# Two-stage attention ahead of two feed-forward stages: the order of an attention turn on all engines, and its crossing into the next stage

## What is computed

```python
def sm_attn(qq, kk, vv):
    s = scale * np.matmul(qq, kk.transpose(0, 1, 3, 2))
    s = s - np.max(s, axis=-1, keepdims=True)
    a = np.exp(s)
    a = a / (np.sum(a, axis=-1, keepdims=True) + 1e-09)
    return np.matmul(a, vv)
p_packed = sm_attn(p, k, v)               # q, k, v: (8, 8, 576, 64), p: (8, 8, 32, 64)
out = sm_attn(q, p_packed, p_packed)
x = out.transpose(0, 2, 1, 3).reshape(4608, 512)
h = x @ w_in                              # 512 x 2048
g = (a0 + a1*h + a2*h**2 + a3*h**3) / (1 + |b0|*|h| + |b1|*h**2 + 1e-6)
y = g @ w_out                             # 2048 x 512
h = y @ w_in2                             # 512 x 1024
solu = h * softmax(h); result = layernorm(solu) * g_ln @ w_out2
```

## Time and profile before

| | us |
|---|---|
| median of 3 runs | 1232.92 (1231.55 to 1236.02) |
| the profiled execution | 1235.92 |
| its span, first to last instruction | 1234.1 |
| TensorE busy in the span | 1180.6 (96%) |
| VectorE, ScalarE, GpSimd busy | 1045.4, 832.8, 437.5 |
| data moved, mean rate | 116 MB, 94 GB/s |

### The profile page before, as it was taken

The page is one execution under the profiler, slowest core; times in us unless marked ns, Lnnn a source line. Parts: engine busy times, 40 slices in busy tenths (PEclk is TensorE's granted clock), DMA queues, the critical chain, the costliest instruction groups (busy, mean ns, idle before and its releaser), DMA issues.

```text
span 1234.1 us, 25214 instructions
## 1 busy us (share of the span) xinstructions
PE 1180.6 (96%) x9824; PEld 1049.5 (85%) x9824; DVE 1045.4 (85%) x1621; ACT 832.8 (67%) x1302; POOL 437.5 (35%) x284
## 2 busy tenths in 40 slices
PE   6788887999999999999999999999999999999998
PEld 3455555999999999999999999997788888888887
DVE  3767778999999999999999999988677687776763
ACT  2456559888888888888888888754555454454543
POOL 1333322334343343333433334354434344353300
PEclk8889889999999999999999999999999999999999
DMA  8779975321202212012121121121121121111211
GB/s 286 226 265 348 333 272 217 105 81 38 81 28 64 81 38 80 29 62 81 43 75 37 55 80 37 54 88 44 43 54 49 36 58 43 51 47 38 60 26 35
DMA packets 70758, 116.25 MB, mean 94 GB/s; under 512 B 9728, under 2 KB 40448, under 8 KB 70656
## 3 DMA queue, kind: packets, MB, share of 16 engines
q1 hardware_dynamic: 70656, 114.85, 28.8%
HBM read 74.46 MB, written 40.37 MB: 93 GB/s over the span
## 4 chain that ended last, share of the span: by engine, by line
PE 90%; DVE 5%; issue 3%; ACT 1%; DMA 1%; POOL 0%; SPq 0%; ACTq 0%; DVEq 0%
PE ps_y L73 11%; PE ps_y L75 11%; PE ps_y L74 11%; PE ps_h L73 6%; PE ps_h L75 6%; PE ps_h L74 6%; PE ps_o L73 5%; PE ps_o L75 5%; PE ps_o L74 5%; PE ps_h L1394 4%; PE ps_h L1395 4%; PE ps_h L1396 4%; PE ps_s L381 3%; PE ps_s L394 3%; PE ps_t L1419 2%
## 5 line engine op out<-in xcount | busy, mean ns | idle before, releaser
L1018 POOL TENSOR_TENSOR den<-den,h_abs 128x576 f32<-128x576 f32 x128 | 222.3, 1737 | 401.6 <-ACT den L971 401.6
L73 PE MATMUL ps_y<-g_hi,wout_hi 128*128 128x288 f32 x1024 | 303.6, 297 | 0.0
L74 PE MATMUL ps_y<-g_lo,wout_hi 128*128 128x288 f32 x1024 | 302.6, 295 | 0.0
L75 PE MATMUL ps_y<-g_hi,wout_lo 128*128 128x288 f32 x1024 | 301.6, 295 | 0.0
L75 PEld LDWEIGHTS ps_y<-g_hi,wout_lo 128*128 128x128 f32 x1024 | 193.0, 188 | 0.0
L74 PEld LDWEIGHTS ps_y<-g_lo,wout_hi 128*128 128x128 f32 x1024 | 192.3, 188 | 0.0
L73 PEld LDWEIGHTS ps_y<-g_hi,wout_hi 128*128 128x128 f32 x1024 | 192.1, 188 | 0.3 <-ACT wp_out L530 0.2
L73 PE MATMUL ps_h<-x_hi,wp_hi 128*128 128x288 f32 x512 | 152.3, 298 | 1.3 <-DVE wp_lo L1033 0.8
L74 PE MATMUL ps_h<-x_lo,wp_hi 128*128 128x288 f32 x512 | 151.3, 295 | 0.0
L75 PE MATMUL ps_h<-x_hi,wp_lo 128*128 128x288 f32 x512 | 150.8, 295 | 0.0
L965 ACT ACTIVATE h_abs<-ps_h 128x576 f32<-128x576 f32 x128 | 83.3, 651 | 82.5 <-PE ps_h L75 82.3
(11 more groups left out here) (164 smaller groups left out, 2594.7 us busy)
## 6 DMA issues: line engine op xcount, KB each, us to landing
wp_scratch<-wp_out SPq DMA_DIRECT2D x32, 512.0 KB, 5.3
wp_lo<-wp_scratch SPq DMA_DIRECT2D x32, 512.0 KB, 4.1
k_main<-in_k SPq DMA_DIRECT2D x16, 576.0 KB, 6.7
q_main<-in_q SPq DMA_DIRECT2D x16, 576.0 KB, 6.0
v_main<-in_v SPq DMA_DIRECT2D x16, 576.0 KB, 5.5
y_scratch<-y_out SPq DMA_DIRECT2D x16, 576.0 KB, 3.4
y_lo<-y_scratch SPq DMA_DIRECT2D x36, 256.0 KB, 3.2
out<-result SPq DMA_DIRECT2D x144, 64.0 KB, 1.7
```

The lines of the kernel that those rows point to most:

```text
L73: pe.matmul(out, lh, rh, start=first, stop=False)
L74: pe.matmul(out, lh, rl, start=False, stop=False)
L75: return pe.matmul(out, ll, rh, start=False, stop=last)
L1018: pool.tensor_tensor(den[s % 3][:, :, :], den[s % 3][:, :, :], h_abs[:, :, :], ALU.mult)\
```

## The change

TensorE's turn i becomes: the v products of group i itself in four pieces (20, 16, 20 and 16 products), the two halves of the scores of packed of i+1 behind the first and the second, the two halves of a job behind the third and the fourth, then q's scores of group i-1, packed of i turned, and the queries of i turned. The wait in the middle of q's scores becomes one for the packed tile; the turned packed tile and the ninth query pair move to other PSUM banks (`turn_pack`, `turn_q8`). `job_at` puts job m into turn m + 4, so twelve lie in turns and four in the crossing. The weights get a second staging buffer; two parts are split ahead of the first turn, and in a turn the split stands at the end. SP loads p and k of two groups first, and its turn becomes k, p, weight part, v, a2, job's store, q. kT and the first query buffer change places in SBUF, so that the first wp block waits for the last scores of packed; the tiles of the rational stage's chain are put into other strips. The crossing is written anew on all engines. Removed lines of the loops are left out below where the new ones replace them all.

```diff
-LAST_JOBS = 5
-PAIR_JOBS = 4
+LAST_JOBS = 4
...
-    m = i - QUAD - 1
+    m = i - QUAD
...
+    kT = sb("kT", [P, RUN, DB, PACK])
+    q_main = [sb("q_main0", [P, RUN, DH])]
+    w_stage = [sb("w_stage0", [P, WI]), sbuf.at("w_stage1", [P, WI], sbuf.area - 4 * WI)]
     p_in = [sb(f"p_in{i}", [P, DH]) for i in range(2)]
     v_main = [sb(f"v_main{i}", [P, RUN, DH]) for i in range(2)]
-    kT = sb("kT", [P, RUN, DB, PACK])
+    q_main += [sb("q_main1", [P, RUN, DH])]
...
+    def turn_pack(i):
+        return ps_turn[:, 1, 0:P] if i < GROUPS - 1 else ps_s2[:, 1, HALF + DH:HALF + DH + P]
+    def turn_q8(i):
+        return ps_turn[:, 0, 0:P] if i < GROUPS - 1 else ps_s2[:, 0, HALF:HALF + P]
...
     def parts_at(i):
-        return [i] if i < 5 else [5, 6] if i == 5 else [i + 1] if i < GROUPS - 1 else []
+        return [0, 1] if i < 0 else [i + 2] if i + 2 < 2 * PARTS else []
+    def w_buffer(n):
+        return w_stage[n % 2 if n < 2 * PARTS - 1 else 0]
...
     def next_w(sp, n):
-        sp.wait_ge(w_lo_done, n)
-        load_w(sp, n)
+        after = n + 2 if n < 2 * PARTS - 3 else n + 1
+        if n != 2 * PARTS - 3 and after < 2 * PARTS:
+            sp.wait_ge(w_lo_done, n + 1)
+            load_w(sp, after)
     def sync(sp, coefficients, first_loads):
         first_chunk, first_block, second_block, last_blocks = first_loads
-        load_p(sp, 0)
-        load_k(sp, 0)
-        load_w(sp, 0)
+        for i in range(2):
+            load_p(sp, i)
+            load_k(sp, i)
+        load_v(sp, 0)
         load_q(sp, 0)
-        load_p(sp, 1)
-        load_k(sp, 1)
-        load_v(sp, 0)
+        for n in range(2):
+            load_w(sp, n)
+        sp.wait_ge(kT_ready, 1)
+        load_k(sp, 2)
+        sp.wait_ge(pT_ready, 1)
+        load_p(sp, 2)
+        load_v(sp, 1)
+        sp.wait_ge(kT_ready, 2)
+        load_k(sp, 3)
+        sp.wait_ge(pT_ready, 2)
+        load_p(sp, 3)
         load_q(sp, 1)
+        coefficients(sp)
         for i in range(GROUPS - 1):
-            if i >= 1 and job_at(i - 1) is not None:
-                store_job(sp, job_at(i - 1))
+            if i + 4 < GROUPS:
+                sp.wait_ge(kT_ready, i + 3)
+                load_k(sp, i + 4)
+                sp.wait_ge(pT_ready, i + 3)
+                load_p(sp, i + 4)
+            elif i + 4 == GROUPS:
+                first_chunk(sp)
+            for n in parts_at(i - 1):
+                next_w(sp, n)
             if i + 2 < GROUPS:
-                sp.wait_ge(kT_ready, i + 1)
-                load_k(sp, i + 2)
-                sp.wait_ge(pT_ready, i + 1)
-                load_p(sp, i + 2)
-                sp.wait_ge(qT_done, i + 1)
-                load_q(sp, i + 2)
-            else:
-                first_chunk(sp)
-            if len(parts_at(i)) > 1:
-                next_w(sp, parts_at(i)[1])
-            wait_for(sp, pack_done, i)
-            load_v(sp, i + 1)
-            if i == 0:
-                coefficients(sp)
-            if i + 2 == GROUPS:
+                sp.wait_ge(pack_done, i + 1)
+                load_v(sp, i + 2)
+            if i + 1 == GROUPS - 1:
                 first_block(sp)
             if i >= 2:
                 store_a2(sp, i - 2)
-            if parts_at(i + 1):
-                next_w(sp, parts_at(i + 1)[0])
+            if job_at(i) is not None:
+                store_job(sp, job_at(i))
+            if i + 2 < GROUPS:
+                sp.wait_ge(qT_done, i + 1)
+                load_q(sp, i + 2)
...
+        def pack(pe, i, part):
+            if part == 0:
                 pe.wait_ge(probs1T_ready, i + 1)
                 pe.wait_ge(v_in[i % 2], 16 * (i // 2 + 1))
-                wait_for(pe, scores2_out, i)
-                wait_for(pe, packT4_lo_ready, i)
-            for t in range(half * PAIRS, (half + 1) * PAIRS):
+                wait_for(pe, scores2_out, i - 1)
+                wait_for(pe, packed_ready, i)
+            for t in range((0, 5, 9, 14)[part], (5, 9, 14, 18)[part]):
                 for h in range(GH):
                     mm = pe.matmul(ps_pack[head(h), :], probs1T[head(h), t, :], v_main[i % 2][head(h), t, :],
                                    start=(t == 0), stop=(t == RUN - 1), skip_group_check=True)
-            if half == 1:
+            if part == 3:
...
                 if h == GH // 2:
-                    pe.wait_ge(packT4_lo_ready, i + 1)
+                    pe.wait_ge(*((packed_ready, i + 2) if i < GROUPS - 1 else (packT4_lo_ready, GROUPS)))
...
+        for c in range(2):
+            scores_of_packed(pe, 0, c)
+        turn_last_pair(pe, 0)
+        turn_queries(pe, 0)
+        for c in range(2):
+            scores_of_packed(pe, 1, c)
+        for part in range(4):
+            pack(pe, 0, part)
+        turn_packed(pe, 0)
+        for i in range(1, GROUPS - 1):
+            pack(pe, i, 0)
+            scores_of_packed(pe, i + 1, 0)
+            pack(pe, i, 1)
+            scores_of_packed(pe, i + 1, 1)
+            pack(pe, i, 2)
+            job_block(pe, i, 0)
+            pack(pe, i, 3)
+            job_block(pe, i, 1)
+            scores_of_q(pe, i - 1)
+            turn_packed(pe, i)
+            turn_last_pair(pe, i)
             turn_queries(pe, i)
         last = GROUPS - 1
+        for part in range(3):
+            pack(pe, last, part)
+        pe.wait_ge(exp1_ready, GROUPS)
+        features(pe, 0)
+        pack(pe, last, 3)
+        job_block(pe, last, 0)
+        job_block(pe, last, 1)
+        scores_of_q(pe, last - 1)
+        pe.wait_ge(wp_act_out, 2 * job_at(last) + 1)
+        features(pe, 1)
+        turn_last_pair(pe, last)
+        turn_packed(pe, last)
+        features(pe, 2)
+        turn_queries(pe, last)
+        features(pe, 3)
+        b, c, d, e = range(JOBS - LAST_JOBS, JOBS)
         last_block(pe, b, 0)
+        scores_of_q(pe, last)
         last_block(pe, b, 1)
+        for m in (c, d, e):
             for n in range(2):
                 last_block(pe, m, n)
...
         def turn_packed(pe, i):
             pe.wait_ge(packed_ready, i + 1)
-            pe.transpose(turn_pack, packed.rearrange("p a d -> p (a d)"), ident[:, :]).then_inc(packT_done, 1)
+            if i == GROUPS - 1:
+                pe.wait_ge(scores2_out, GROUPS - 1)
+            else:
+                wait_for(pe, packT4_lo_ready, i)
+                if job_at(i) is not None:
+                    pe.wait_ge(wp_act_out, 2 * job_at(i) + 1)
+            pe.transpose(turn_pack(i), packed.rearrange("p a d -> p (a d)"), ident[:, :]).then_inc(packT_done, 1)
...
-            pe.wait_ge(*((qT8_out, i + 1) if n == 0 else (qT_out, i + 1)))
+            if n == 0:
+                pe.wait_ge(qT8_out, i)
+                pe.wait_ge(packT4_lo_ready, i)
+            else:
+                pe.wait_ge(qT_out, i)
...
+        first_terms(act, 0)
+        for n in parts_at(-1):
+            weights_high(act, n)
         for i in range(GROUPS - 1):
             if i == 3:
                 next_coefficients(act)
+            first_terms(act, i + 1)
             if job_at(i) is not None:
                 job_to_sbuf(act, job_at(i), 0)
                 job_to_sbuf(act, job_at(i), 1)
+            if i == GROUPS - 2:
+                break
+            if i == 0:
+                last_pair_to_sbuf(act, i)
+                qT_to_sbuf(act, i)
+                act.wait_ge(zeros, 1)
+            packT_to_sbuf(act, i)
             if i >= 1:
                 second_terms(act, i - 1)
+                last_pair_to_sbuf(act, i)
+                qT_to_sbuf(act, i)
+            for n in parts_at(i):
+                weights_high(act, n)
         last = GROUPS - 1
+        a, b, c, d, e = range(job_at(last), JOBS)
         early["x_hi"](act, 0)
+        packT_to_sbuf(act, last - 1)
+        last_pair_to_sbuf(act, last - 1)
+        second_terms(act, last - 2)
         early["block_hi"](act, 0)
+        qT_to_sbuf(act, last - 1)
+        early["block_hi"](act, 1)
+        act.wait_ge(w_lo_done, GROUPS)
+        act.wait_ge(pT_ready, GROUPS)
+        act.wait_ge(probs1T_ready, GROUPS)
+        early["head"](act, 0)
         job_to_sbuf(act, a, 0)
         job_to_sbuf(act, a, 1)
+        act.wait_ge(pack_done, GROUPS)
+        early["reciprocal"](act, 0)
+        second_terms(act, last - 1)
+        early["head"](act, 1)
+        last_pair_to_sbuf(act, last)
+        packT_to_sbuf(act, last)
+        qT_to_sbuf(act, last)
+        early["head"](act, 2)
         job_to_sbuf(act, b, 0)
+        early["reciprocal"](act, 1)
         job_to_sbuf(act, b, 1)
+        early["block_hi"](act, 2)
         job_to_sbuf(act, c, 0)
+        early["head"](act, 3)
         job_to_sbuf(act, c, 1)
+        second_terms(act, last)
         job_to_sbuf(act, d, 0)
+        early["reciprocal"](act, 2)
         job_to_sbuf(act, d, 1)
         job_to_sbuf(act, e, 0)
         job_to_sbuf(act, e, 1)
...
+        row_max(dve, 0)
+        turn_keys(dve, 1)
+        turn_probs1(dve, 0)
         for i in range(GROUPS - 1):
```

(31 more changed lines are left out.)

191 lines of the change are left out of this document (52 added, 139 removed).

## The result

The changed kernel takes 1237.33 us (median of 9 runs, 1234.09 to 1240.04) beside 1232.63 us for the kernel before (9 runs, 1229.89 to 1236.02): ratio 1.0038, 95% interval 1.0021 to 1.0054. It is slower by 0.4%, less than the 0.5% named ahead, and 16 us from the predicted 1221.4. Its profiled execution took 1240.04 us, the slowest of the nine, with a span of 1238.2. One later execution of the kernel before was in a slow state, 2318.79 us, and counts in no ratio.

The account below looks back on a forecast made before the run. TensorE was taken as the bound from 216 us on, so only the first ps_y product's start could move: 26.0 + 28.2 + 109.0 + 41.3 = 204.5 against 216.0, 11.5 us less, giving 1221.4 us; range 1214 to 1226, chance 0.50.

Parts of the forecast that it names:

- Start: Time to the third row maximum (group 2): 26.0 us instead of 30.0, bounds 24.6 to 27.
- Ten turns: From the row maximum of group 5 to that of group 15: 109.0 us instead of 116.9, 10.9 a turn.
- 6.2 us for a block: Arrival time of 256 TensorE instructions, from two blocks in 12.48 us; 1.6 blocks make 9.9 us a turn.
- the floor of 10.4 us from the data: Least time of a turn with a job: its 3.67 MB on the DMA engines at some 354 GB/s.
- neither allows a turn under 9.0: VectorE's 8.2 us of work a turn and TensorE's 9.3 less its wait, taken as the shortest turn with jobs.
- The pieces: V products of a turn in four pieces: a gain of 0.4 us a turn, bounds 0 and 1.3.
- Three turns: Turns before all have jobs, between the maxima of groups 2 and 5: 28.2 us instead of 31.6, 1.5 blocks each.
- Crossing: Last row maximum to first ps_y product: 37.5 + 3.2 (extra work) + 0.6 (new waits) = 41.3 us, bounds 38 and 45.
- The signs: Trace marks named ahead: third maximum, turn lengths, DMA share of 0.95, gaps at multiples of 126 loads, crossing 40 to 43 us.
- D: Rival: second exponentials ahead of ScalarE's query copies make TensorE's jobs wait as long as today's gaps; 1233 us, chance 0.08.
- A: Rival: burstier loads in the ten turns hold code up, turns of 12.8 us; 1240 us, chance 0.12.
- C: Rival: turns gain little, at 11.5 us, and a crossing of 43 takes half back; 1229 us, chance 0.22.

Follow-up runs that it names:

- a_act: Kernel after with ScalarE's split of the second wp block moved behind the head of step 0 and a job's two copies: 1237.91 us, ratio 1.0035 to the kernel before.
- a_late: Kernel after with SP's q and weight issues spread, second wp block split later, step 3's head and step 2's reciprocal behind the last job's copies: 1236.98 us.
- a_spread: Kernel after with SP issuing q and the weight part behind the next turn's scores of packed: 1236.02 us, ratio 1.0019 to the kernel before.
- a_norm_half_v: Kernel after without the second half of each group's v products, GpSimd's division moved ahead of the weight part's low half: 1206.21 us.
- a_whole: Kernel after with the four pieces of v products in one run again, then scores of packed, then the job's halves: 1278.24 us, ratio 1.035 to the kernel before.
- a_half_v: Kernel after with the second half of each group's v products left out, 72 of 144 a turn: 1212.34 us.
- b_pad: Kernel before with 40 matmuls and 40 weight loads more a turn, repeats of the first v product of each half: 1236.49 us in one run.

## Why the prediction was wrong

**What bounds the kernel: right.** The time moved by what ps_y moved, 4.1 us in the profiles (1240.04 against 1235.92), and the rest stayed to a hundredth. The kernel became slower where 11.5 us less were forecast.

**Start: right.** 26.92 us against 26.0, in the bounds of 24 to 27. The reason held too: the block is late inside group 1's v products, at 22.08 us instead of 21.35. The other versions with all v products in pieces took 23.6 to 25.6 us, so the hit within a microsecond is in part luck.

**Ten turns: the largest miss, 7.8 us.** Three steps of the sum failed. First, *6.2 us for a block* was a mean, and I multiplied it by 1.6 blocks a turn to say that code allows 9.9. A mean says nothing here: a turn's blocks aren't spent evenly, and only the quick ones meet an arrival that is longer than they last. The prediction gave "half a microsecond for blocks that come late"; the kernel after waits 17.6 us in the ten turns, 1.8 a turn, and runs slowly behind waits such as the one shown above. Second, *the floor of 10.4 us from the data* came from a mean rate of 343 GB/s that was no limit (why the rate was lower there isn't shown; waits of TensorE that hold loads back would do it); the runs put it near 9.0. The 10.9 a turn was this floor and half a microsecond, so it rested on two wrong terms. Third, *"neither allows a turn under 9.0"* counted each engine's work alone. The new ring through GpSimd, 9.73 us, is longer than the 9.3 of the earlier trace rows; the change shows it (a weight part's high half now stands at a turn's end on ScalarE, and on GpSimd its low half stands ahead of the division), and I followed VectorE's and TensorE's lists but not GpSimd's.

**The pieces: wrong in size by far.** I took 0.4 us a turn, bounded by 1.3, since the densest block "passes in 3.6 us instead of 3.0". Taking the cuts away costs 41 us in the new order, about 3 a turn. The bound was the waits of the kernel before, and in that kernel the queries between the two halves of v were a cut already. What the new order had to be compared with was itself without the cuts. So the four pieces are no gain over the kernel before; they keep the new order from a loss.

**Three turns: missed by 3.1 us.** The failed step is the same mean of 6.2 us for a block; 31.34 us are 10.4 a turn, at a clock of 0.89, with late blocks in them. With nearly no loads they are 27.3 (9.1 a turn, clock 1.00), near the 9.4 forecast.

**Crossing: right in kind, short by 3.8 us, and 0.08 over the upper bound of 45.** ScalarE in order of time:

```profile
189.44 1.15 ACT L1001 ACTIVATE wp_hi<-wp_lo 128x512 fp32r<-128x512 f32 x2 [2.99 <-DMA wp_lo<-wp_scratch]
...
217.19 1.02 ACT L573 ACTIVATE wp_out<-ps_s 128x1024 f32<-128x1024 f32 x1 [0.83 <-PE ps_s L382]
```

TensorE, at the start and at the end of the crossing:

```profile
177.12 0.63 PE L410 MATMUL ps_s<-v_main,probs1T 32*32 32x64 f32 x26 [2.08 <-issue]
...
217.08 0.61 PE L72 MATMUL ps_h<-x_hi,wp_hi 128*128 128x288 f32 x1
...
220.13 0.41 PE L72 MATMUL ps_y<-g_hi,wout_hi 128*128 128x288 f32 x1
```

ScalarE's last copy ends 43.2 us after the last maximum, against 37.5 before (214.97 + 1.01). It is busy 35.55 us instead of 33.31. It waits 2.99 us for the second wp block, which I had as hidden at 4.5 us for a landing and which was issued at 183.14 and used at 189.44, and 1.83 us through a late block at the start. From 189.44 to the last copies it hardly waits. Behind its last copy come 1.9 us that didn't exist before: the features products end the crossing at a granted clock of 0.50, 1.2 GHz (0.24 us apart, 3.05 us in all), where the earlier trace rows had ps_y 0.06 us after the copy. Moving the wait for the wp block (a_act) left the crossing at 44.5; taking 3.9 us from ScalarE's list (a_late) gave 3.2. From the first head on ScalarE's list is the length, as the constant 27.5 to 27.7 us show, and this part isn't longer than in the kernel before (28.9). The loss lies around it: the first head begins 15.45 us after the last maximum instead of 8.56, and 1.9 us come behind the last copy. So the sum's term of 3.2 + 0.6 us put the wait for the wp block, the late block and the slow clock at nothing; the share of each was read from the profile and not tested by itself.

**The signs.** Waits at multiples of 126 loads, three of them at other products than v's, came as forecast. Turns of 9 to 10 us before the jobs (10.4), turns of 10.4 to 11.4 with them (11.7) and a DMA share of 0.95 (0.84) did not, and the crossing passed the 45 us that were to prove the prediction wrong.

**Rivals.** The total is D's, 1233 with turns as now, plus a crossing 3 us worse; its stated reason (TensorE's jobs wait for query copies) isn't in the trace: in the ten turns TensorE waits for no copy of ScalarE's. The reason is A's without its size: blocks behind data, at 11.7 us a turn and not 12.8; that the loads became burstier isn't shown, since spreading them (a_spread) gained 1.3 us. I had given the two 0.20 together. C had the crossing right in kind.

The Trainium skill, "Runtime: NRT & Kernel Launch", section "Instruction fetch mechanics", holds that fetching is mostly hidden. Here it is hidden where matmuls are long: behind ps_y, before the change and after it, no wait of TensorE is without a semaphore. Among 32x64 products it isn't: with all products and loads the ten turns wait 9 to 38 us for code, and with half of the v products 0 to 2.7.

## What to carry to other kernels

Where TensorE waits and no semaphore accounts for it, look at what it ran just ahead: many tiny products use up a block of code faster than the next arrives, and spreading them among longer ones can be worth more (41 us here) than the waits that an order removes. See whether each such wait ends behind a packet of the instruction queue. Never bound that cost by the mean time of a block: try the same products in another order, which keeps the number of blocks, and halve the tiny products to see what is left. For a new order follow every engine's list around the whole ring, the least busy engine's too, before giving a shortest turn; and work pushed behind a deadline is owed to the next one, so measure the stretch behind it as well.

## What the runs showed of the hardware

- TensorE's waits without a semaphore depend on how densely small products stand (17.6 us in ten turns with 144 in four pieces, 38.2 with the same 144 in a row) and on the data in flight (38.2 us against 20.3, with the DMA engines at 0.70 and 0.36), and not simply on the number of instructions: 80 more a turn cost about 2 us.
- Each of them ends 1.2 to 1.7 us (one 0.7) behind the end of a 16 KB packet of the instruction queue (188 waits in 20 profiles).
- The DMA engines carried 392 GB/s over 91 us with all of this kernel's transfers, and 407 to 410 in single turns (a_norm_half_v); the 343 GB/s of the earlier trace rows was no limit.
- After a wait of 2.72 us TensorE ran at 1.2 GHz: eight products took 2.19 us instead of 1.19. The ten turns of a_whole, with 38.2 us of such waits, had a mean grant of 0.87, those of a_half_v 1.00. But b_pad had 0.99 with 13.6 us of them, the kernel before 0.90 with 14.4.
